# A matrix LSTM attention and two dense layers on one core: looped program with transposes on PE, or unrolled program with stacked inputs from the host

## The reference, cut to what matters

```python
for t in range(S):
    m_new = np.maximum(f_gate[:, :, t] + m, i_gate[:, :, t])
    f_stab = np.exp(f_gate[:, :, t] + m - m_new)
    i_stab = np.exp(i_gate[:, :, t] - m_new)
    m = m_new
    C = f_stab[..., None, None] * C + i_stab[..., None, None] * einsum('bhd,bhe->bhde', vt, kt)
    n = f_stab[..., None] * n + i_stab[..., None] * kt
    denom = np.maximum(np.abs(einsum('bhd,bhd->bh', n, qt)), 1.0)[:, :, None]
    y[:, :, t] = sigmoid(o_gate[:, :, t]) * einsum('bhde,bhe->bhd', C, qt) / denom
x = y.transpose(0, 2, 1, 3).reshape(B * S, H * D)
x = np.maximum(x @ w_in1, 0) ** 2 @ w_out1
h = x @ w_in2
out = np.where(h > 0, h, np.exp(np.minimum(h, 0)) - 1) @ w_out2
```

## Time and profile before

| what | us |
|---|---|
| median of 3 runs | 949.78 |
| lowest and highest run | 947.1, 955.18 |
| span of the profiled execution | 941.4 |

### The profile page before, as it was taken

How to read it: one execution, slowest core, us unless ns; L and a number is a source line. 1 busy time by engine, 2 the same in 40 slices (tenths; PEclk the granted TensorE clock), 3 DMA queues, 4 the chain that set the end, 5 groups by cost and what they waited for, 6 DMA issues and landing times.

```text
span 941.4 us, 18105 instructions
## 1 busy us (share of the span) xinstructions
PE 915.3 (97%) x6170; PEld 895.8 (95%) x6170; DVE 504.0 (54%) x866; ACT 453.0 (48%) x932; POOL 408.7 (43%) x497
## 2 busy tenths in 40 slices
PE   5899999999999999999999999999999999999998
PEld 5788999999999999999999999999999999999998
DVE  5499955556545646455556466444444444444443
ACT  2455646545454545455465465444444444444443
POOL 3445544444444545554444342434343433434333
PEclk7799999999999999999999999999999999999999
DMA  6255311111111212211110133000000000000000
GB/s 117 56 101 136 68 29 29 29 30 29 29 30 29 43 18 44 42 29 29 29 30 1 55 108 86 1 22 1 23 1 22 1 22 0 21 0 22 1 22 21
DMA packets 122072, 33.05 MB, mean 35 GB/s; under 512 B 102280, under 2 KB 121736, under 8 KB 121992
## 3 DMA queue, kind: packets, MB, share of 16 engines
q1 hardware_dynamic: 121992, 32.00, 16.3%
HBM read 28.05 MB, written 3.93 MB: 34 GB/s over the span
## 4 chain that ended last, share of the span: by engine, by line
PE 87%; DVE 8%; issue 2%; ACT 1%; DMA 1%; POOLq 0%; POOL 0%; SPq 0%; DVEq 0%; ACTq 0%
PE hps L1039 36%; PE acc L1053 34%; PE att L947 4%; PE att L962 3%; PE att L973 2%; PE att L991 1%; PE att L933 1%; PE att L940 1%; PE att L968 1%; DMA x<-in_i_gate 1%; DVE wout L712 1%; DVE win L705 1%; PE att L955 1%; DVE win L706 1%; PE hps L1011 1%
## 5 line engine op out<-in xcount | busy, mean ns | idle before, releaser
L1053 PE MATMUL acc<-wout,ghi 128*128 128x320 f32 x1536 | 349.0, 314 | 3.9 <-DVE glo L845 1.6
L1039 PE MATMUL hps<-xth,win 128*128 128x384 f32 x1280 | 350.2, 338 | 2.5 <-DVE xtl L823 2.0
L1053 PEld LDWEIGHTS acc<-wout,ghi 128*128 128x128 f32 x1536 | 257.2, 188 | 9.7 <-issue 5.5
L1039 PE MATMUL hps<-xtl,win 128*128 128x384 f32 x768 | 259.9, 338 | 0.0
L1053 PE MATMUL acc<-wout,glo 128*128 128x320 f32 x768 | 237.1, 309 | 0.0
L1039 PEld LDWEIGHTS hps<-xth,win 128*128 128x128 f32 x1280 | 228.4, 188 | 3.1 <-DVE xtl L823 2.2
L523 POOL TENSOR_TENSOR glo<-gfull,ghi 128x384 fp32r<-128x384 f32 x128 | 130.2, 1017 | 218.3 <-ACT ghi L671 218.3
L505 POOL TENSOR_TENSOR gfull<-act_tmp 128x384 f32<-128x384 f32 x128 | 106.8, 835 | 173.8 <-ACT act_tmp L640 173.0
L640 ACT ACTIVATE act_tmp<-hps 128x384 f32<-128x384 f32 x128 | 62.9, 492 | 179.9 <-PE hps L1039 179.6
L845 DVE TENSOR_TENSOR glo<-gfull,ghi 128x384 fp32r<-128x384 f32 x128 | 81.6, 638 | 121.2 <-POOL gfull L505 120.8
L1039 PEld LDWEIGHTS hps<-xtl,win 128*128 128x128 f32 x768 | 144.7, 188 | 0.0
(11 more groups left out here) (172 smaller groups left out, 981.9 us busy)
## 6 DMA issues: line engine op xcount, KB each, us to landing
q_t<-in_q SPq DMA_DIRECT2D x23, 160.0 KB, 2.9
k_t<-in_k SPq DMA_DIRECT2D x23, 160.0 KB, 3.3
o_t<-in_o_gate SPq DMA_DIRECT2D x23, 160.0 KB, 3.5
v_t<-in_v SPq DMA_DIRECT2D x23, 160.0 KB, 3.5
x<-in_w_out SPq DMA_DIRECT2D x16, 160.0 KB, 2.5
out_x<-x SPq DMA_DIRECT2D x16, 160.0 KB, 1.8
x<-in_w_in SPq DMA_DIRECT2D x16, 128.0 KB, 2.2
in<-in_w_in SPq DMA_DIRECT2D x16, 128.0 KB, 2.3
```

What stands on the lines that cost most here:

```text
L1039: last = nc.tensor.matmul(hps[j % 2][:, 0:NT], win[:, j, w, :], x[:, kk, :], start=(i == 0), stop=(i == len(parts) - 1))
L1053: last = nc.tensor.matmul(acc[u][:, 0:DM], g[j % GR][:, cols], wout[:, j, w, :], start=(j == 0 and i == 0), stop=(j == NF - 1 and i == 2))
```

## The change

The program is rewritten with the same dense arithmetic and the same blocks and slots, with all loops unrolled.

- Tiles go chunk by chunk over the batches (tile g is chunk g // 4 of batch g % 4), so a block of 384 tokens has tiles of three batches, and the state of a batch is needed four tiles later. The output rows are placed accordingly.
- The host gives q and k transposed and already stacked to 120 rows of 8 x 128 values (`qk`, one DMA of 120 x 8 KB a tile), k, v with its column of ones, and o in one array (`kvo`, one DMA of 0.50 MB), and each weight slice in one array (`w_all`). The transposes of q and k on PE and their copies on ACT go. ACT rounds the stack (`split_hi_qk`, 1024 values a partition, twice), POOL subtracts for q (40 partitions x 1024), DVE for k (40 x 1024).
- The running maximum of each row is stored to DRAM, and each tile loads its 8 x 128 values broadcast to 128 partitions (0.52 MB) straight into `wts`; ACT makes the exponents with eight activations of 128 columns (scale -1, bias a). The products L968 and `pick` go. POOL masks before the product with the scores, in one instruction, and takes wv from the last column of the weights.
- The state is spread to 120 rows by four SBUF to SBUF DMAs (`load_state`); the products L955 go. ACT rounds it, DVE subtracts.
- A tile still has five slots, but with other parts: on PE part 0 is the scores, part 1 the update and the product with the state, part 2 the weights times v, part 4 the transposes of x of the same tile. DVE: weigh; update and gate + 1; sum with the state and gate reciprocal; sum, denominator, x and a small copy (part 3); split of k, x_lo and split of the state (part 4).
- The row pass runs on 32 partitions, with one scan over all chunks and a short one over their ends. Two weight slices instead of six are split before the first block, ring of three instead of six. POOL splits all of w_out. x of layer 2 is transposed from where it lies, with a copy of its last 64 columns alone.

The core of the diff; behind SP's lists stand, in this order, what POOL does behind gfull of a slot, ACT behind relu and ghi, DVE behind glo, and PE between the first product of slot t and the second of slot t - 2:

```diff
-        FIRST = [(0, 0), (1, 0), (0, 1), (0, 2), (1, 1), (1, 2), (0, 3), (0, 4), (2, 0), (1, 3), (2, 1), (0, 5), (2, 2),
...
+        def tile_at(block, j):
+            u, part = divmod(j, PERIOD)
+            if block >= BLOCKS - 1 or u >= T:
+                return None, None
+            return T * (block + 1) + u, part
...
+            def load_m(g):
+                wait(sp, "m_stored" if g < B else "m_rest_stored", 16)
+                wait(sp, "intra_ps", g - 2)
+                src = m_dram[chunk_of(g), heads_of(g), :].rearrange("r t -> (r t)").unsqueeze(0).broadcast_to([P, HT])
+                sp.dma_start(wts[g % 3][:].rearrange("p h t -> p (h t)"), src).then_inc(m_in[g % 3], 16)
+            def load_qk(g):
...
+                wait(sp, "q_lo", last + 1)
+                wait(sp, "k_lo", last + 1)
+                sp.dma_start(raw_of(g), qk[g]).then_inc(s["qk2_in" if g in (1, 3) else "qk_in"], 16)
+            def load_state(g):
+                n = with_state(g)
+                wait(sp, "state_ready", g - B + 1)
+                wait(sp, "st_lo", n)
...
+                for first, count, d in parts_of_rows():
+                    sp.dma_start(dst[first:first + count, :], src[d:d + count, :]).then_inc(s["state_in"], 16)
...
+                    if part == 0 and g + 2 < TILES and g + 2 > 4:
+                        load_m(g + 2)
+                    if part == 1 and B <= g + 1 < TILES:
+                        load_state(g + 1)
+                    if part == 2 and g + 1 < TILES and g + 1 > 3:
+                        load_kvo(g + 1)
+                    if part == 4 and 4 < g + 2 < TILES:
+                        load_qk(g + 2)
...
+                            if part == 2:
+                                mask(g + 1)
+                                if g + 1 < TILES - B:
+                                    make_wv(g + 1)
+                            if part == 3:
+                                split_q_lo(g + 1)
...
+                            if part == 0 and more:
+                                out_gate(g + 1) if g + 1 > 3 else None
+                                exponents(g + 1, 0)
+                            if part == 1 and more:
+                                exponents(g + 1, 1)
+                            if part == 2 and more:
+                                split_hi_qk(g + 1, 0)
+                            if part == 3 and more:
+                                split_hi_qk(g + 1, 1)
+                            if part == 4:
+                                x_hi(g, (block + 1) % 2, g % T, A2)
+                                if more and g + 1 >= B:
+                                    split_state_hi(g + 1)
...
+                            if part == 0:
+                                weigh(g)
+                            if part == 1:
+                                update_state(g)
+                                if more:
+                                    gate_plus(g + 1)
+                            if part == 2:
+                                add_inter(g)
+                                if more:
+                                    gate_recip(g + 1)
+                            if part == 3:
+                                add_intra(g)
+                                finish(g)
+                            if part == 4:
+                                if more:
+                                    split_k_lo(g + 1)
+                                x_lo(g, (block + 1) % 2, g % T, A2)
+                                if more and g + 1 >= B:
+                                    split_state_lo(g + 1)
...
+                        if part == 0:
+                            scores(g)
+                        if part == 1:
+                            state_added(g)
+                            from_state(g)
+                        if part == 2:
+                            within(g)
+                        if part == 4:
+                            x1_transposed(g)
```

More of the change, by code:

```diff
@@ L21 @@
-from collections import namedtuple
 from contextlib import ExitStack
@@ L75, in mlstm_two_dense_layers @@
         x2 = sb("x2", [P, TILES, DM])
-        x1 = [sb(f"x1_{i}", [P, DX]) for i in range(2)]
         xth = [sb(f"xth_{i}", [P, 3, NT], F32R) for i in range(2)]
@@ L120, in mlstm_two_dense_layers @@
[L120 to L129 removed]
+        a_col = sb("a_col", [P, CH, R])
@@ L295, in run @@
[L295 to L306 removed]
+            used_before = len(range(i, NF, RING))
@@ new lines, in _ @@
+            sp.dma_start(rows[:, 0:2, :], gates).then_inc(s["gates_in"], 16)
+            load_qk(0)
+            load_kvo(0)
+            load_qk(1)
+            load_kvo(1)
+            wait(sp, "m0_row_ready", 1)
+            sp.dma_start(m_dram[0], m_run[:, 0:P]).then_inc(s["m_stored"], 16)
+            load_m(0)
+            load_m(1)
+            load_m(2)
+            load_qk(2)
+            for n in range(RING):
+                load_w(n)
+            wait(sp, "m_row_ready", 1)
+            sp.dma_start(m_dram[1:CH].rearrange("c r t -> r c t"), by_chunk[3][:, 1:CH, :]).then_inc(s["m_rest_stored"], 16)
@@ new lines, in _ @@
+            load_m(3)
+            load_kvo(3)
+            load_qk(4)
+            load_m(4)
+            for block in range(BLOCKS - 1):
+                for j in range(NF):
+                    g, part = tile_at(block, j)
+                    if block == 0 and j + RING < NF:
+                        load_w(j + RING)
+                    if g is None:
+                        continue
+                    if part == 0 and g + 2 < TILES and g + 2 > 4:
[6 more added lines that the diff above has]
+                        load_qk(g + 2)
@@ L382, in _ @@
+            wait(sp, "intra_ps", TILES)
+            for n in range(NF, 2 * NF):
+                load_w(n)
+            for i in range(TILES):
+                u = i % T
+                g = i
+                row = batch_of(g) * S + chunk_of(g) * P
+                wait(sp, "acc_free", TILES + i + 1)
+                sp.dma_start(out[row:row + P, :], out_stage[u]).then_inc(out_done[u], 16)
             for u in range(T):
@@ new lines, in out_gate, with exponents @@
+            def out_gate(g):
+                kvo_loaded(act, g)
+                wait(act, "x_ready", g - 1)
+                nc.scalar.activation(gate[g % 2][:], o_of(g), ACT.Exp, scale=-1.0).then_inc(s["egate_ready"], 1)
+            def exponents(g, u):
+                c, b = chunk_of(g), batch_of(g)
+                w = wts[g % 3]
+                if u == 0:
+                    act.wait_ge(m_in[g % 3], 16 * (g // 3 + 1))
+                    act.wait_ge(s["a0_col_ready" if c == 0 else "col_ready"], 1)
+                for h in range(u * HH, (u + 1) * HH):
+                    r = b * H + h
+                    nc.scalar.activation(w[:, h, :], w[:, h, :], ACT.Exp, bias=a_col[:, c, r:r + 1], scale=-1.0)\
+                        .then_inc(s["exp_ready"], 1)
@@ new lines, in _ @@
+            last.then_inc(s["col_ps"], 1)
+            keep_warm(8)
+            scores(1)
+            keep_warm(12)
+            state_added(0)
+            within(0)
+            scores(2)
+            x1_transposed(0)
+            state_added(1)
+            within(1)
+            x1_transposed(1)
+            pe.wait_ge(s["int_exp"], 1)
+            pe.wait_ge(s["hsum_ready"], 1)
+            for c in range(1, CH):
+                last = nc.tensor.transpose(A0[:, (c - 1) * R:c * R], f_sum[:, c * P:(c + 1) * P], ident[0:R, 0:R])
@@ L1082, in after_layer @@
-            def after_layer(layer):
-                if layer == 2:
-                    for j in range(NF - LAG, NF):
-                        second_product(2, PAIRS - 1, 1, j)
-            run(pe, block, after_layer)
+                    t = NF * block + j
+                    if j == 0 and block > 0:
+                        second_product(t - LAG)
+                    first_product(t)
+                    g, part = tile_at(block, j)
+                    if g is not None:
+                        if part == 0:
[7 more added lines that the diff above has]
+                            x1_transposed(g)
```

1402 lines of the change are left out of this document (589 added, 813 removed).

## The result

The changed kernel takes 1060.67 us (median of 4 runs, 1056.29 to 1061.96), the kernel before 949.34 us in the same comparison (947.1 to 955.18). The ratio is 1.1175, 95% interval 1.1112 to 1.1237: slower by 111 us. In all comparisons, runs over 1.5% above the fastest of the same kernel are left out. The profiled execution has a span of 1057.7 us, 116.3 more than before; the median of the runs lies 3.0 us above it, not 8.4 as before.

What follows compares the result with a forecast made beforehand. PE, busy 97% of the span, was taken to bound the kernel before. Opening 50, seven blocks 527, block 0 extra 5 and third stage 411.5 gave 993.5 us span; with 8.4 more, 1002 us, range 938 to 1043.

Steps and rivals of the forecast that it cites:

- rival A: The main forecast: slots go as predicted, PE waiting for x in each tile, about 1002 us; chance 0.60.
- the opening: Stretch before the first dense product: that product at about 50 us instead of 71.2, saving 21 us, bounds 10 and 28.
- block 0: First block of layer 1: weight slices wait on SP behind attention loads, 5 us more, between 0 and 12.
- the third stage: Last block of layer 1 and all of layer 2: unchanged at 411.5 us, 0, at most 2 either way.
- The wait for x in part 4: PE's transposes of x, one slot behind DVE's finish: PE idles 4.35 us, a tile takes 23.05.
- The split of q: POOL's subtraction of 1024 elements behind its square in part 3: 2.4 us, holding DVE's glo as long.
- The transfer at the head of ACT's queue: ACT's output gate waits for kvo, landing 7.2 us after slot 0; a tile then takes 23.75 us.
- The clock: Idle gaps halve PE's clock: the two products behind the wait take 4.7 us instead of 2.7, a tile 25.1.
- The mean tile: Average time of an attention tile in layer 1: 24.2 us, so a block takes 75.3 us.
- Rival B: DVE and POOL turns go well, kvo in time, no low clock: tiles 20.3 to 20.9, 920 to 933 us; chance 0.17.
- the later slot 0 gives ACT's transfer time: With the low clock, a tile's later slot 0 lets kvo land in time, so x stays ready at 19.95 us.
- Rival D: Transfers bind: kvo and qk 2 us later a tile, block 0 by 12, tiles of 25.8, 1043 us; chance 0.15.

Runs made afterwards that it cites:

- e9: e8 with POOL's split of q moved from behind the square of part 3 to the end of part 2: 895.14 us.
- e8: e7 with the edits of e3 and e6 added: 929.46 us, median of four runs, ratio 0.9789 to the kernel before.
- e3: The changed kernel with five places instead of three for the weights of layer 2: 1034.22 us.
- e6: The changed kernel with each weight slice of block 0 issued by SP one slot earlier: 1063.84 us.
- e7: The changed kernel with the edits of e1 and e2, and k rounded and split in part 1 instead of parts 3 and 4: 958.33 us.
- e10: e9 with DVE's w_in remainders of block 0 moved behind its attention steps: 891.36 us.
- e11: e10 with DVE's split of k of tile 2 ahead of the finish of tile 0: 891.29 us, four runs, ratio 0.9403 to the kernel before.
- e1: The changed kernel with the transposes and splits of x one slot later: 1066.46 us.
- e2: The changed kernel with kvo issued one tile earlier, ahead of qk and the state transfers: 1050.92 us.
- e4: The changed kernel with twenty dummy products on PE before its wait for x: 1054.82 us.

## Why the prediction was wrong, point by point

The sign was right, rival A as to its mechanism; the size was not: 1002 us with a range up to 1043, and 1060.67 measured. The span was to be 993.5 and is 1057.7, so 64 us are missing. By the table above they are 12 in the opening, 15 in block 0, 12 in blocks 1 to 6, and 22 and 4 behind them (1 us too many, since the stages are not cut at quite the same places). Without the 26 behind them the time would have been 1035 us, inside the range: the step that failed most is the third stage, put at nothing.

**What held.** PE's own work in a tile, 18.6 us: in e9 the products with v come 18.4 to 18.5 us apart. The wait for x in part 4: idle of 4.1 to 6.4 us before the transposes, where 4.35 was said. The split of q: 2.37 us on average for 2.4. The transfer at the head of ACT's queue: in the tile behind the one shown the gate starts at 349.63, 7.5 us after the relu of slot 0 (342.11), for 7.2; over the second and third tiles of blocks 1 to 6 it is 6.2 to 8.6. The clock: the product behind the wait at half speed, 0.73 for 0.46. The mean tile, 24.4 for 24.2. Rival B's condition, a finish within 4.9 us of slot 3, was not met: in blocks 1 to 6 x is ready 6.7 to 7.6 us after the start of slot 3's relu, and 4.7 only in the last tile. The turn-taking: the split of q held glo to 308.29, 0.43 us behind its own end (307.86). The Trainium skill, SBUF — State Buffer, "Who interferes with whom", says that a VectorE instruction with two SBUF inputs contends with a GpSimd one that reads SBUF, as an exclusive lock; the trace agrees. e8 goes beyond one instruction, with a glo of 3.52 us behind two of POOL.

**The third stage, "0, at most 2 either way": 26, the largest miss.** I counted its products and its splits, and not its transfers. The three places were there before; what is new is that one transfer waits for both halves. This and the distance between the halves stand in the program, and the landing time could have been bounded from the trace of before. What had to be asked was how long one round is: issue, landing, split on ACT, remainder on POOL, next issue. e3 shows it (40.5 for 62.4 us, and 365.4 for 370.6 in layer 2).

**Block 0, "5 us more, between 0 and 12": 18 over the mean of the other blocks (95.6 for 77.3).** The step named was not the one. I put the excess on slices that wait on SP; e6 issued them earlier and gained nothing. The excess over the other blocks was 11.5 in e7 (76.3), 17.2 in e9 (75.6) and 13.7 in e10 (72.1), where DVE's remainders were moved: those are 3.5 of it. For some 14 us no run here has an answer. In the trace of e10 they stand in slots 5, 10 and 15 of block 0 (10.7, 8.7 and 8.2 us, against 3.9, 3.9 and 4.6 in block 1), where PE waits for DVE's sum and for x. In the first of them DVE's 8-element step takes 1.88 us (0.17 in the same place of e9's block 3) while POOL goes from a square to a split of w_out and on to the next square:

```profile
82.19 1.88 DVE L603 SCALAR_TENSOR_TENSOR den<-hsum 128x8 f32<-128x8 f32 x1
```

Block 0 makes 13 such splits (three slices are split ahead of it, not two). That they are the cause is a reading and was not run.

**The opening, "first product at about 50": 62.36.** Up to the exponents of tile 2 the count was right (36 said, 35.8 in the trace). Then three tiles go through DVE in series. DVE of the changed kernel:

```profile
37.98 0.20 DVE L612 COPY x<-x 128x64 f32<-128x64 f32 x1
...
49.80 0.20 DVE L612 COPY x<-x 128x64 f32<-128x64 f32 x1
...
53.10 0.63 DVE L552 TENSOR_TENSOR wts<-wts,acc 128x512 f32<-128x512 f32 x1
...
60.04 0.20 DVE L612 COPY x<-x 128x64 f32<-128x64 f32 x1
```

The weighing of tile 2 comes at 53.10, by program order behind the finish of tile 1, 17 us after its exponents; I had it done by 44. Each tile takes 10 to 12 us from one finish to the next, weighing, products, finish, and from 40 us on PE runs at its lower level: the windows from 40 to 50 and from 50 to 62 us show a granted clock of 0.50, with PE busy for 6.99 of 10 and 7.35 of 12 us. That this series is the cause is read from the trace; e11, the one run on it, moved one small step of it, for 1.5 us.

**The tile.** Its mean was right (24.4 for 24.2), by a sum that was not built right, so in part by luck. I put the wait for x, the transfer and the clock in a row: 23.05, 23.75, 25.1. They are chains side by side that cross in the split of k: DVE's finish sets x and, one glo behind it, k; k frees `raw`, for which SP's whole queue waits, kvo last; kvo releases ACT, whose relus lead to the finish. So the step "the later slot 0 gives ACT's transfer time" failed: the transfer starts behind the same late finish. The pairs show it: e1 +6, e2 -10, e4 -6, e1 and e2 together -39, with the split of k -102. By the prediction's sum, in which the wait for x ends last, e1 alone would have brought most of it. The extra 12 us of blocks 1 to 6 are 2 a block, 1.4 of them in the sixteenth slot (4.1 us in block 3, not 2.7).

**The clock as a step of its own, "the tile takes 25.1".** The Trainium skill, TensorE: Matmul & The Clock Gate, "Part 1: The HAM clock gate", says that PE stands at half its clock by default and that activity releases it; the granted clock of 0.50 from 310 to 313 us, behind an idle time of 5.11 us, agrees. The price was set too high: the second and the first product behind the wait took 3.8 us (311.08 to 314.85), where 4.7 was said and 2.7 is the time at full clock. And in e4 the mean clock came back from 0.913 to 0.954 and the kernel by 6 us, none of it in blocks 1 to 6: a slow product costs only where PE sets the end.

**Rival D** (transfers bind, 1043 us, 0.15) was nearest in time, and half right: transfers do bind, but by their place in a queue and by what they wait for. Their volume does not, since the same bytes pass in tiles of 18.4 us in e9. The DMA share of the stage was 0.31 (0.20 in the earlier trace rows), and not above the 0.35 that was named as a sign for the forecast itself.

## What to carry to other kernels

When a change puts a wait into a loop, follow it all the way round to itself, the DMA queue included: each round has a length, the slowest sets the beat, and removing one of two equal rounds shows little, so try them together before either is called harmless. Merging two transfers into one saves issues, but the place is then free only behind the last reader of both parts. A ring of buffers is safe only if one round of it (issue, landing, every reader, next issue) is shorter than the steps that it covers; where it is not, each step costs the difference. A long instruction on POOL belongs beside a DVE step that it does not stretch, as the reciprocal here, and not between a square and the subtraction that waits for it.

## What the runs showed of the hardware that was not expected

- Four pieces of the state, 157.5 KB in all (52.5 the largest), hold SP for 2.92 us, 0.73 each, while an issue of 0.98 MB for qk takes 0.36: on this queue the number of transfers cost more than their size. I had taken 0.5 for each.
- A DVE subtraction with two inputs in SBUF can lose to two POOL instructions in a row: 3.52 us for 0.56 (e8). Behind one, the split of q, it took 2.37 for 0.29 (block 0).
- An idle time of 5.11 us cost little speed. The windows of the changed kernel around the tile shown (columns as in the earlier trace rows) have the lower level from 310 to 313 us and the full one from 314 on:

```profile
310.00:313.00 3.00, 2.47 (x10) 2.48 (x11) 2.87 (x6) 0.86 (x2) 0.00 (x0) 0.50 0.00 0
...
314.00:316.00 2.00, 2.00 (x14) 2.00 (x13) 0.00 (x0) 0.92 (x2) 0.39 (x1) 1.00 0.91 242
```
